# Softmax gates moved from the routing stage into the attention loop of a fused attention and mixture-of-experts kernel

## The reference, cut to what matters

```python
# 1. attention with decay: B=2, H=8, S=768, D=64; lam near 0.97..0.99 per head
for b in range(nb):                          # blocks of 64
    intra = (q_b @ k_b.T * Dmask) @ v_b
    inter = (q_b * lam_pow) @ kv_state
    out_b = intra + inter
    kv_state = lam**64 * kv_state + (k_b * rev_pow).T @ v_b
x = out.transpose(0, 2, 1, 3).reshape(1536, 512)

# 2. mixture of experts, one expert of E=8 per token
logits = x @ w_gate                          # 1536 x 8
expert_idx = argmax(logits, axis=1)
probs = exp(logits - logits.max(-1))
probs /= probs.sum(-1) + 1e-9
gate_w = probs[arange(N), expert_idx]
for e in range(8):
    xe = x[expert_idx == e]
    out[expert_idx == e] = gate_w * (relu(xe @ w1[e]) @ w2[e])

# 3. second network
h = out @ w_in; g = h - tanh(h); result = g @ w_out
```

## Time and profile before

| | us |
|---|---|
| median of three runs | 547.7 (543.15 to 550.82) |
| the profiled execution's own time | 547.09 |
| its span, first to last instruction | 545.2 |
| TensorE busy | 509.8 (94%) |
| VectorE busy | 367.3 (67%) |
| GpSimd busy | 319.4 (59%) |
| ScalarE busy | 257.4 (47%) |

### The profile page before, as it was taken

One profiled execution on the slowest core, in us unless ns is written; L12 is line 12 of the kernel. 1 busy time (PEld: TensorE's weight loads), 2 busy tenths in 40 slices (PEclk: granted clock), 3 DMA queues, 4 the chain that ended last, 5 costly groups with the idle time before them and its releaser, 6 DMA issues.

```text
span 545.2 us, 10842 instructions
## 1 busy us (share of the span) xinstructions
PE 509.8 (94%) x3948; PEld 452.5 (83%) x3949; DVE 367.3 (67%) x513; ACT 257.4 (47%) x467; POOL 319.4 (59%) x263
## 2 busy tenths in 40 slices
PE   5999748799999999999999999999999999999994
PEld 4899648799999999999888888888888888888883
DVE  7333266756546455364379999989987774998781
ACT  1222316466656566476455454545444434443431
POOL 4766046635454444445368988986855554875553
PEclk9999969899999999999999999999999999999998
DMA  8878426465667757767280000000100000100002
GB/s 312 319 274 291 164 66 200 155 204 175 234 206 215 232 189 231 215 206 232 74 298 1 1 0 1 1 1 20 59 0 1 1 1 0 60 20 1 0 1 77
DMA packets 32410, 64.55 MB, mean 118 GB/s; under 512 B 3697, under 2 KB 7793, under 8 KB 32369
## 3 DMA queue, kind: packets, MB, share of 16 engines
q1 hardware_dynamic: 30448, 57.71, 32.2%
q0 software_dynamic: 1920, 6.29, 3.5%
HBM read 57.69 MB, written 6.29 MB: 117 GB/s over the span
## 4 chain that ended last, share of the span: by engine, by line
PE 85%; DVE 4%; DMA 4%; issue 3%; ACT 2%; POOL 1%; SPq 1%; ACTq 0%; DVEq 0%; POOLq 0%
PE bank L318 25%; PE bank L320 25%; PE bank L319 24%; DMA wst<-in_w_dram 3%; PE bank L1156 2%; PE bank L1131 2%; PE bank L1142 2%; PE bank L1178 1%; PE bank L1242 1%; PE bank L1185 1%; PE bank L1168 1%; DVE x_sorted L1031 1%; POOL out_dram L650 1%; ACT x_h L742 1%; DMA x_sorted<-token_rows,tokid 1%
## 5 line engine op out<-in xcount | busy, mean ns | idle before, releaser
L608 POOL TENSOR_TENSOR w_l<-wst,w_h 128x512 fp32r<-128x512 f32 x64 | 84.5, 1321 | 105.7 <-ACT w_h L713 105.7
L658 POOL TENSOR_SCALAR big<-h_sq 128x512 uint8<-128x512 f32 x48 | 80.3, 1673 | 37.3 <-ACT h_sq L797 37.0
L671 POOL TENSOR_TENSOR g_l<-g,g_h 128x512 fp32r<-128x512 f32 x48 | 63.9, 1330 | 45.5 <-ACT g_h L807 45.5
L318 PE MATMUL bank<-wo_h,g_h 128*128 128x512 f32 x192 | 75.4, 393 | 0.0
L320 PE MATMUL bank<-wo_l,g_h 128*128 128x512 f32 x192 | 75.1, 391 | 0.0
L319 PE MATMUL bank<-wo_h,g_l 128*128 128x512 f32 x192 | 74.6, 389 | 0.0
L320 PE MATMUL bank<-x_l,win_h 128*128 128x512 f32 x188 | 74.3, 395 | 0.0
L318 PE MATMUL bank<-x_h,win_h 128*128 128x512 f32 x188 | 73.9, 393 | 0.0
L319 PE MATMUL bank<-x_h,win_l 128*128 128x512 f32 x188 | 73.7, 392 | 0.0
L318 PE MATMUL bank<-xs_h,w_h 128*128 (+1 forms) x256 | 70.9, 277 | 2.6 <-issue 1.4
L318 PE MATMUL bank<-h_h,w_h 128*128 128x232 f32 x256 | 71.6, 280 | 1.5 <-DVE h_l L1021 1.3
(11 more groups left out here) (159 smaller groups left out, 1098.5 us busy)
## 6 DMA issues: line engine op xcount, KB each, us to landing
wst<-in_w_dram SPq DMA_DIRECT2D x128, 256.0 KB, 3.9
qk_in<-in_qk_t_dram SPq DMA_DIRECT2D x12, 512.0 KB, 6.1
kv_in<-in_kv_dram SPq DMA_DIRECT2D x12, 512.0 KB, 5.2
win<-in_w_in_dram SPq DMA_DIRECT2D x8, 512.0 KB, 4.5
wo<-in_w_out_dram SPq DMA_DIRECT2D x8, 512.0 KB, 8.0
token_rows<-x_sb SPq DMA_DIRECT2D x12, 256.0 KB, 3.4
x_sorted<-token_rows,tokid POOLq DMA_INDIRECT x12, 4.6
out_dram<-rows,tokid POOLq DMA_INDIRECT x12, 3.0
```

What stands on the lines that cost most here:

```text
L318: pe.matmul(dst, lh, rh, start=start, stop=False, skip_group_check=True)
L608: pool.tensor_tensor(w2_l[:, j % STG], wst2[:, j % STG], w2_h[:, j % 2].bitcast(F32), ALU.subtract).then_inc(w2l_ready, 1)
L658: pool.tensor_scalar(big[:, f % 2], h_sq[:, f % 2], T * T, None, ALU.is_ge).then_inc(big_ready, 1)
L671: pool.tensor_tensor(g_l[:, f % 2], g[:, f % 2], g_h[:, f % 2].bitcast(F32), ALU.subtract).then_inc(gl_ready, 1)
```

## The change

The gates are formed tile by tile in the attention loop and x is scaled in place in `x_sb` ahead of its store. The logits are written into the scores' banks. The shifted logits of all tiles are there at the end of the loop. The gathered rows are turned as they come. The gate's split, its spreading, its products and its sum go, as do the scalings in expert 0; `keep_awake` has 18 products in place of 8.

```diff
+        def psG(t):
+            return psS[(t + 1) % 2][:, 0, 0:E]
...
             def store_x(t):
-                sp.wait_ge(x_ready, t + 1)
+                sp.wait_ge(gated, t + 1)
                 sp.dma_start(x_dram.ap()[in_tile(t):in_tile(t) + P], x_sb[:, t % UN]).then_inc(x_stored[t % UN], 16)
...
+            def exps(t):
+                act.wait_ge(logit_ready, t + 1)
+                act.activation(logit_exp[:, t, :], logit_shift[:, t, :], ACT.Exp).then_inc(exp_ready, 1)
+            def gate_x(t):
+                act.wait_ge(gate_ready, 2 * t + 2)
+                act.mul(x_sb[:, t % UN, :], x_sb[:, t % UN, :], gate[:, 1, t:t + 1]).then_inc(gated, 1)
             for t in range(NT):
                 if t:
                     x_t(t - 1)
+                if t > 1:
+                    exps(t - 2)
+                if t > 2:
+                    gate_x(t - 3)
                 x_out(t)
             x_t(NT - 1)
-            act.wait_ge(route_step, 2)
-            act.activation(logit_exp[:], logit_shift[:], ACT.Exp).then_inc(exp_ready, 1)
+            exps(NT - 2)
+            gate_x(NT - 3)
+            exps(NT - 1)
+            gate_x(NT - 2)
+            gate_x(NT - 1)
...
             def logits(t):
                 dve.wait_ge(logits_done, t + 1)
-                dve.tensor_copy(logit[:, t, :], psG).then_inc(logit_ready, 1)
+                dve.tensor_reduce(logit_max[:, t:t + 1], psG(t), AX.X, ALU.max).then_inc(max_ready, 1)
+                dve.wait_ge(max_ready, t + 1)
+                dve.tensor_scalar(logit_shift[:, t, :], psG(t), logit_max[:, t:t + 1], None, ALU.subtract).then_inc(logit_ready, 1)
+            def gates(t):
+                dve.wait_ge(exp_ready, t + 1)
+                dve.tensor_reduce(exp_sum[:, t:t + 1], logit_exp[:, t, :], AX.X, ALU.add).then_inc(sum_ready, 1)
+                dve.wait_ge(sum_ready, t + 1)
+                dve.tensor_scalar(gate[:, 0, t:t + 1], exp_sum[:, t:t + 1], 1e-9, None, ALU.add).then_inc(gate_ready, 1)
+                dve.wait_ge(gate_ready, 2 * t + 1)
+                dve.reciprocal(gate[:, 1, t:t + 1], gate[:, 0, t:t + 1]).then_inc(gate_ready, 1)
...
                 if t + 1 < NT:
                     masked(t + 1)
+                if t > 1:
+                    gates(t - 2)
                 if t:
                     logits(t - 1)
                 if t < NT - B:
                     state_step(t)
+            gates(NT - 2)
             logits(NT - 1)
...
-            dve.tensor_reduce(logit_max[:], logit[:], AX.X, ALU.max).then_inc(route_step, 1)
-            dve.tensor_tensor(logit_shift[:], logit[:], bc(logit_max), ALU.subtract).then_inc(route_step, 1)
...
-            dve.tensor_reduce(exp_sum[:], logit_exp[:], AX.X, ALU.add).then_inc(gate_step, 1)
+            gates(NT - 1)
...
-            dve.tensor_copy(gate_p[:, 0], gate[:]).then_inc(gate_step, 1)
...
-            dve.tensor_tensor(gate_s[:], gate_s[:], psGate[:, 2], ALU.add).then_inc(gate_s_ready, 1)
...
             def scores(t):
                 ge(pe, sm_ready, t - 1)
+                ge(pe, logit_ready, t - 2)
...
             def x_transposes(t):
                 pe.wait_ge(x_ready, t + 1)
                 ge(pe, xT_ready, t)
-                ge(pe, logit_ready, t)
...
-            for t in range(NT):
-                i = pe.matmul(psGate, in_row[:, t], gates[:, t], start=t == 0, stop=t == NT - 1)
-            i.then_inc(gate_done, 1)
-            keep_awake(pe, 8)
+            keep_awake(pe, 18)
             def turn(tiles):
                 for t in tiles:
-                    scaled_wait(pe, t)
+                    pe.wait_ge(gathered[t], 16)
...
-            scale(range(2))
-            if first: scale(LATER[j])
```

More of the change, by code:

```diff
@@ L92, in decay_attention_moe_kernel @@
         tokid = sb("tokid", [P, NT], U32)
-        gate_s = sb("gate_s", [P, NT])
         off_i = sb("off_i", [1, E], I32)
@@ L154, in decay_attention_moe_kernel @@
         exp_sum = sb("exp_sum", [P, NT], at=small_mem)
-        gate = sb("gate", [P, NT], at=small_mem)
+        gate = sb("gate", [P, 2, NT], at=small_mem)
         place_f = sb("place_f", [P, NT], at=small_mem)
@@ L231, in decay_attention_moe_kernel @@
         logits_done = sem("logits_done")
+        max_ready = sem("max_ready")
         logit_ready = sem("logit_ready")
+        gate_ready = sem("gate_ready")
+        gated = sem("gated")
         route_step = sem("route_step")
         exp_ready = sem("exp_ready")
+        sum_ready = sem("sum_ready")
         places_done = sem("places_done")
-        scaled_v = sem("scaled_v")
-        scaled_s = sem("scaled_s")
         one_hot_ready = sem("one_hot_ready")
         above_ready = sem("above_ready")
-        gate_step = sem("gate_step")
         row_ready = sem("row_ready")
@@ L298, in decay_attention_moe_kernel @@
         psO, psX = bank[:, 4:6, 0:PAIRS * D], bank[:, 6, :]
-        psU, psG = bank[:, 7, 0:PAIRS * D], bank[:, 6, 0:E]
+        psU = bank[:, 7, 0:PAIRS * D]
+        def psG(t):
+            return psS[(t + 1) % 2][:, 0, 0:E]
         halves = [(0, slice(0, D)), (1, slice(D, P))]
@@ L306, in decay_attention_moe_kernel @@
         psId = bank[:, 2, 0:2 * NT].rearrange("p (v a) -> p v a", v=2)
-        psGate = bank[:, 3, 0:3 * NT].rearrange("p (v a) -> p v a", v=3)
         psYs = [bank[:, b:b + 2, :].rearrange("p b (a t) -> p (b a) t", a=2)[:, :, 0:WIN] for b in (4, 6)]
@@ L721, in _ @@
             w2_high(0, 0)
[L723 to L727, removed]
             def take(tiles):
@@ L753, in expert @@
                     hidden(j, unit)
-                    if first:
-                        scale(LATER[j])
                     if not (last and j + 2 >= JT):
@@ L957, in _ @@
                               ALU.is_le).then_inc(route_step, 1)
-            dve.wait_ge(route_step, 8)
+            dve.wait_ge(route_step, 6)
             dve.tensor_reduce(col[:], past_col[:, :, 1:], AX.X, ALU.add).then_inc(route_step, 1)
-            dve.wait_ge(route_step, 9)
+            dve.wait_ge(route_step, 7)
             dve.scalar_tensor_tensor(row[:], col[:], -float(P), place_f[:], ALU.mult, ALU.add).then_inc(row_ready, 1)
@@ L973, in _ @@
             mark_rows(0, 4)
-            dve.wait_ge(route_step, 10)
+            dve.wait_ge(route_step, 8)
             dve.tensor_tensor(ids[:, :, 0], in_col[:], tile_no[:], ALU.mult)
@@ L978, in _ @@
                 mark_rows(t, t + 4)
-            dve.wait_ge(gate_step, 1)
-            dve.tensor_scalar(gate[:], exp_sum[:], 1e-9, None, ALU.add).then_inc(gate_step, 1)
             dve.wait_ge(id_done, 1)
             dve.tensor_copy(tokf[:], psId[:, 1]).then_inc(route_step, 1)
-            dve.wait_ge(route_step, 11)
+            dve.wait_ge(route_step, 9)
             dve.scalar_tensor_tensor(tokf[:], psId[:, 0], float(P), tokf[:], ALU.mult, ALU.add).then_inc(route_step, 1)
-            dve.wait_ge(route_step, 12)
+            dve.wait_ge(route_step, 10)
             dve.tensor_copy(tokid[:], tokf[:]).then_inc(tokid_ready, 1)
-            dve.wait_ge(gate_step, 2)
-            dve.reciprocal(gate[:], gate[:]).then_inc(gate_step, 1)
             dve.tensor_copy(off_i[:], psPos[0:1, 0, :])
-            dve.wait_ge(gate_step, 3)
-            dve.tensor_copy(gate_p[:, 0], gate[:]).then_inc(gate_step, 1)
[L992 to L1004, removed]
-            counts()
[L1006 to L1010, removed]
-            dve.tensor_tensor(gate_s[:], gate_s[:], psGate[:, 2], ALU.add).then_inc(gate_s_ready, 1)
-            dve.wait_ge(gate_s_ready, 1)
+            counts()
             def w1_low(j, unit):
@@ L1025, in _ @@
             w1_low(1, 1)
[L1027 to L1032, removed]
             def take(tiles):
@@ L1184, in gate_logits @@
                     for half, cols64 in halves:
-                        j = pe.matmul(psG[cols64], x_T[:, t % 2, i, cols64], w_gate_sb[:, i, :], start=i == 0,
+                        j = pe.matmul(psG(t)[cols64], x_T[:, t % 2, i, cols64], w_gate_sb[:, i, :], start=i == 0,
                                       stop=i == KT - 1, skip_group_check=True)
```

24 lines of the change are left out of this document (5 added, 19 removed).

## The result

The changed kernel took 563.44 us (median of 4, 562.8 to 564.43); the ratio to the kernel before is 1.0347 (95% interval 1.0296 to 1.0397): slower by 3.5%, where 555.8 with a range of 547 to 562 was forecast, and no change beyond 2% was given 0.72. The ratio is taken from fast executions alone; the medians of all, 563.44 and 548.23, lie 2.8% apart. The profiled execution took 562.8 us.

What follows compares the result with a forecast made beforehand. TensorE, busy 509.8 of 545.2 us, was taken as the bound. Loop +11.2, clock in it +3.4, routing -0.8 and first expert -5.1 made +8.7 on 547.1: 555.8 us, range 547 to 562.

Steps and rivals of the forecast that it cites:

- I let two of the four drop the clock, at 1.7 us each ... +3.4.: Attention loop: two of four 3.4 us TensorE stalls drop the clock to half speed, costing +3.4 us.
- rival (a): Attention loop: every stall drops the clock for most of the pass, 2.9 us each; 564.0 us in all; chance 0.2.
- The stated bound, +6.8: Attention loop: clock loss if all four stalls drop the clock, +6.8 us, more if it stays low longer.
- The late loads: Attention loop: loads queued behind the delayed store of x arrive late and end the loop 11.2 us later.
- T+2.25: Attention loop: store and following loads issue 2.25 us after T, the start of a pass's transposes, landing 6.2 us later.
- Every second pass: Attention loop: every second pass stands 3.4 us for its load; the pass after finds its load there.
- The moved wait: Attention loop: the store waits for the gated x, three passes later than before, with loads behind it in SyncE's queue.
- Added beside other work, at nothing: Attention loop: the operations added to VectorE (some 0.8 us) and ScalarE (0.9 us) per pass cost no time.
- Routing and first gathers: Stage between attention loop and first expert product: shorter chain, more keep-awake products; -0.8 us, bounds -1.3 and +0.2.
- First expert: First expert: removing scalings saves 5.1 us (stall 3.5, clock 1.3, gather 0.3); 3.7 if `w1_low(6)` is held.
- (b): Attention loop: load bursts land faster, 5.2 us, stalls are 2.4 us without clock drops; 548.4 us; chance 0.27.
- (c): Attention loop: the moved store doesn't hold up the loads, so only gains remain, -5.9 us, 541.2 us; chance 0.08.

Runs made afterwards that it cites:

- 6: Kernel before, gates unmoved, with each store of x held until two unread ScalarE copies, three passes later, are done: 561.68 us, ratio 1.0303.
- 1: Changed kernel with the store of tile t-7 in place of that of t-4, so no loop load stands behind an unready store: 541.65 us, ratio 0.997.
- 2: Kernel before with only the store's wait moved, to ScalarE's copy of the transposes three passes later: 553.71 us, ratio 1.0181.
- 5: Kernel before, unchanged, profiled once more on the chip of the other runs: 545.92 us.
- 9: Changed kernel, unchanged, run again on another chip: 562.15 us, ratio 1.0357.
- 7: Changed kernel with the scaling of tile t-3 put first in ScalarE's pass, ahead of the copy of the transposes: 548.41 us, ratio 1.011.

## Why the prediction was wrong

**The step that failed: "I let two of the four drop the clock, at 1.7 us each ... +3.4."** Measured: +10.7 by the passes, and 9.6 less in the kernel with filled stalls. Three of four dropped, and both factors were short. The price was read from one window of the first expert (1.3 us), where the clock was back after about 3 us; in the loop the half clock lasted for the rest of the pass and ran into the next, so one drop cost 3.2 to 4.3 us, and 6.3 where it lasted two passes (6: T(7) to T(9) took 17.13 us, less 2 x 4.53 and a stall of 1.82). And rival (a) let the drop begin at stalls of "some 3.3 us"; it came at 2.79, 2.34, 2.14 and 1.82. The stated bound, +6.8 "and more if the clock stays low longer", had the reason in it and not the number. With 10.7 in place of 3.4 the sum is 563.1, beside the measured 562.8; that it comes so near is luck, since the other terms were off by -2.5 (late loads), +1.7 (routing), -0.2 (first expert) and +1.0 (behind it).

**The late loads** (+11.2): right in mechanism and place, 8.7 measured. T+2.25 was T+1.95, the first three landings took 6.5, 6.0 and 6.5 (forecast 6.2), the last 5.2. The four stalls come to 11.1 us where 13.6 were forecast; 2.4 us of gaps in the profile before go under in both counts. The store is issued about two and a half passes later than before (from T-0.28 to T+1.95 two passes on), not three; the forecast's landing times don't use the three. "Every second pass" is exact in the chain.

**The moved wait as cause, not the work:** shown by 1 (work without the wait: no loss), and by 2 and 6 (wait without the work: loss). "Added beside other work, at nothing" holds: passes of 4.53 us in version 1, but for one wait of 0.38 us.

**Routing and first gathers** (-0.8, bounds -1.3 and +0.2): +0.9, outside the bounds. T(11) to the end of the products that give the token numbers took 14.02 us for 12.97: the way to the one-hot choice is 0.3 shorter and `past_col` 0.3 shorter, but the held `row` added 1.1, and the products for the places, of which the 12 long ones ran at half clock (0.99 for 0.54), 0.65 together. The way from there to the first product was only 0.2 shorter, though a scaling of 0.72 left it: the keep-awake products, ending at 100.58, held the transposes in its place. That GpSimd's first subtraction shifts against VectorE's chain was a step not taken: I followed VectorE's chain only.

**First expert** (-5.1): -5.3. The stall and the short clock loss behind it went; `w1_low(6)` took the place, as named, and was free after 3.19 us instead of the 4.9 (99.0 to 103.9) behind the gain of 3.7. The fills hold the scaling, which has one input (3.02 us without them for 4.6), and not the subtraction, which has two (3.23 without them for 3.22). This agrees with the rule of the Trainium skill, SBUF — State Buffer, section Who interferes with whom, that only GpSimd instructions which read SBUF hold a two-input operation.

**Rivals.** (a), given 0.2, came nearly as it stood: 564.0 against 562.8, by terms that partly cancel: late loads 2.5 and clock 0.9 us too high, the gains of routing and first expert 1.5 too high as well, and 1.0 us behind the first expert that it doesn't have. (b), faster landings, came true for the last burst only. (c) is out. The range of 562 was cut short of (a), which was the second error: the two ends of an unknown with a steep effect both belonged in it.

**Open.** The profile of version 1 is 5.2 us shorter than that of the kernel before in 5, on another chip (539.0 for 544.2), 4.7 of it in the first expert, but the ratio of version 1 is only 0.997. The single runs of the kernel before beside it reach from 539.0 to 548.67, so the stall may be missing in some executions; this is a guess. In 6, which has the same first expert, no scaling was over 1.10 us; of the kernel before itself no profile here shows such a one. Nor is it settled why one stall of about 2 us drops the clock and another doesn't.

## What to carry to other kernels

In a queue that issues in order, a wait is a wait for all that stands behind it: moving a store's condition by about two and a half passes moved two loads that had nothing to do with it. Let stores trail until their wait is already met; here that brought the ratio from 1.035 to 0.997, some 20 us. Where a change makes TensorE stand again and again, price the stall with the slow work behind it: in this loop 11.1 us of stalls brought 10.7 of half clock, and cheap products in the gaps brought the ratio from 1.035 to 1.014, some 11 us, though the stores and the loads behind them were held as before.

## What the runs showed of the hardware that was not expected

- The granted clock fell to 0.50 behind stalls of 1.82, 2.06, 2.14 and 2.34 us (experiments 6 and 9) and stayed full behind 1.78 (2), 2.06 (profile after) and 2.11 (6). Around two microseconds in this loop it goes one way or the other, and the length of the stall alone doesn't decide: in 6 it stayed full behind 2.11 and fell behind 1.82.
- Once down, it came back at the end of the pass, in the next or at the end of the next, some 7 us (the third drop of the profile after) to 15 us (9, from 52.42 to 67.9), though TensorE had no pause in it (windows at 8.00 of 8.00 busy and 0.50).
- VectorE was held until GpSimd had finished several instructions issued back to back: 4.59, 4.63 and 4.62 us for a scaling of 0.5 us (the kernel before, 2 and 5). A single GpSimd subtraction holds an operation on 12 columns as long: 1.26 us for 0.17.
- A load of 512 KB takes SyncE 0.4 us to issue, and now and then 1.0 to 1.95 (1.06 in the profile after, 1.95 in 7, there with a stall and a drop of the clock behind it).
